# Down projections of the later pairs with the weights stationary and 512 tokens moving

## The chip, the cores and the metric

The kernel runs on one core of a Trainium2 chip. The metric is device time in microseconds (us), from the runs of the whole program; a profiled execution gives the span, from the first to the last instruction, and the times of each engine: PE (the matrix engine, with weight loads shown apart as PEld), DVE (vector), ACT (scalar), POOL (GpSimd) and SP (which here only issues DMAs).

## The reference

Chunked attention over 4 x 768 tokens gives x with 3072 rows of 512. Then come two feed-forward layers:

```python
def _moe_ref(x, w_a, w_b, w_out):
    a = x @ w_a
    b = x @ w_b
    return (a * b @ w_out).astype(np.float32)

def _moe2_ref(x, w_gate, w1, w2):
    logits = x @ w_gate
    P = np.exp(logits - logits.max())
    for _ in range(8):
        P /= P.sum(1, keepdims=True) + 1e-09
        P /= P.sum(0, keepdims=True) + 1e-09
        P *= N / E
    for e in range(E):
        h = np.maximum(x @ w1[e], 0.0)
        out += P[:, e:e + 1] * (h @ w2[e])
```

N is 3072 tokens, D 512, E 8 experts, w1[e] is 512 x 1024. The gate P is never negative. All data is float32.

## The kernel before, in words

Matmuls run in the fp32r format. Each operand is split into a high part and the rest (the low part), and three matmuls (high x high, high x low, low x high; PARTS) make one float32 product. Activations lie transposed in Y: 128 rows of the model dimension, 4 blocks of them, and the tokens along the free dimension.

Tokens are worked in 3 pairs of two 512-token blocks. The second layer's hidden units are cut into 32 slices of 256, so a pair has 32 units; u counts units over the pairs, 0 to 95, and the later pairs are u = 32 to 95 (k = u - 32). In each unit the up projection (x @ w1) is one 2 x 2 block product by Strassen's method in Winograd's form: 7 products (up(), L891, pos 0 to 6) of 6 matmuls each, 512 tokens moving. Its four results meet as sums: ACT copies a partial sum from PSUM (copy_u, copy_v, L1237 and L1241), DVE adds (sum_22, sum_21, L1515 and L1520).

The first pair's down projection (down(), L968) is plain: 8 groups of 6 matmuls, 512 columns. For the later pairs the down projection is itself a Winograd product (down_product(), L994, q = 0 to 6; DOWN gives for each q the operand H, the block of W2 and the PSUM pair). The hidden block is cut into A11, A12, A21, A22 (tokens by hidden units). ACT applies Relu to each (L1397, L1407, L1413, L1419), POOL makes the four sums S1 to S4 (hidden_sum(), L748 to L760), ACT makes the high parts of the seven operands (hidden_hi(), L1363) and POOL their low parts (hidden_lo(), L765). In down_product() H is the stationary operand and W2 moves, 256 columns at a time: 12 matmuls per q and unit. DVE adds each 128 x 256 result to Y, times the token's gate, which is a scalar of the partition (add_blocks(), L1580), so from then on Y of these pairs holds tokens along the partitions.

PE alternates: up(u, 0), down_product(u - 1, 0), up(u, 1), down_product(u - 1, 1) and so on. The order on each engine is written out by hand in one loop per engine, and each engine runs its list strictly in order. The waits are on semaphores: h_lo (low parts done), z_acc (adds done, which frees PSUM), c_ba (ACT's copy of product 0 into the other PSUM pair, L1370), r_rl (Relu done). SP loads per unit the blocks of W2 (fetch_blocks(), L514 and L515, double buffered) and W1 (fetch_up(), L491, double buffered), and stores the middle pair's 8 tiles in unit 67 (store(), L525). At the start of each pair the seven operands X of the up products are built from Y by ACT (L1191), DVE (L1475 to L1489) and POOL (L683) between the rest.

## Time and profile before

| | us |
|---|---|
| runs | 2695.83, 2698.10, 2700.66 (median 2698.1) |
| profiled execution | 2698.84 |
| its span | 2697.1 |
| PE busy | 2620.4 (97%) |
| POOL busy | 1578.0 (59%) |
| DVE busy | 1501.9 (56%) |
| ACT busy | 1121.4 (42%) |

The chain of work that ended last lies on PE for 89% of the span: 44% on L891, 23% on L994, 18% on L968. Busy time of PE is the time in which a matmul was under way; matmuls overlap, so what one costs is the distance of the starts in the timeline, not the duration shown. Idle time of another engine only costs where PE waits for it.

### The profile page before, as it was taken

The numbers are of one execution on the slowest core, as the hardware profiler recorded it, in microseconds if no ns is written. First come the engines' busy times: TensorE is split into PE (matmuls) and PEld (weight loads), VectorE is DVE, ScalarE is ACT, GpSimd is POOL, SyncE is SP. The second block draws the span as 40 slices with busy tenths as digits, with TensorE's granted clock in tenths as the row PEclk, the third lists the DMA queues.
The fourth block names the chain that finished last, engine by engine and source line by source line (L and its number), as shares of the span: only waits on it lengthen the run. The fifth ranks groups of instructions, "written<-read, shape, count | busy, mean of one in ns | idle before, by whom it ended". The sixth has DMA issues, their size and how long they took to land.

```text
span 2697.1 us, 44988 instructions
## 1 busy us (share of the span) xinstructions
PE 2620.4 (97%) x17568; PEld 2260.8 (84%) x17568; DVE 1501.9 (56%) x2807; ACT 1121.4 (42%) x1957; POOL 1578.0 (59%) x1304
## 2 busy tenths in 40 slices
PE   7879999999999999999999999999999999999999
PEld 6668878878777888888888999999998999999998
DVE  3454454454558555555565555555556555555555
ACT  4544332232333343343344444444445444444443
POOL 0045520010276777777766776767769767677676
PEclk9989999999999999999999999999999999999999
DMA  7746544334355666656646554554544645445453
GB/s 173 164 145 223 200 186 157 152 140 158 132 222 200 245 228 260 253 223 257 258 195 237 188 211 170 192 191 173 210 165 169 242 167 196 187 172 211 165 207 126
DMA packets 184498, 522.37 MB, mean 194 GB/s; under 512 B 55264, under 2 KB 119520, under 8 KB 165088
## 3 DMA queue, kind: packets, MB, share of 16 engines
q1 hardware_dynamic: 184288, 519.50, 52.8%
q8 instruction: 140, 2.29, 0.3%
q14 instruction: 70, 0.57, 0.1%
HBM read 359.02 MB, written 160.50 MB: 193 GB/s over the span
## 4 chain that ended last, share of the span: by engine, by line
PE 89%; DVE 4%; POOL 2%; issue 2%; ACT 1%; DMA 1%; SPq 1%; POOLq 0%; DVEq 0%; ACTq 0%
PE bank L891 44%; PE bank L994 23%; PE bank L968 18%; PE bank L814 2%; POOL X L683 1%; PE bank L853 1%; DVE tmp L1523 1%; PE bank L829 1%; POOL H L765 0%; DMA W<-w_kept 0%; PE bank L841 0%; DMA Qr<-in_q_dram 0%; DVE hid L1700 0%; ACT X L1191 0%; DVE Y L1475 0%
## 5 line engine op out<-in xcount | busy, mean ns | idle before, releaser
L891 PE MATMUL bank<-X,W 128*128 128x512 f32 x5550 | 1413.0, 393 | 18.6 <-ACT tmp L1241 5.8
L891 PEld LDWEIGHTS bank<-X,W 128*128 128x128 f32 x5550 | 1015.3, 189 | 219.5 <-issue 22.5
L1580 DVE SCALAR_TENSOR_TENSOR Y<-bank,gate,Y 128x256 f32<-128x256 f32 x1504 | 623.1, 477 | 413.4 <-PE bank L994 411.9
L994 PEld LDWEIGHTS bank<-W2n,H 128*128 128x128 f32 x5376 | 703.0, 191 | 43.0 <-POOL H L765 4.1
L994 PE MATMUL bank<-W2n,H 128*128 128x256 f32 x5376 | 714.9, 283 | 4.9 <-ACT bank L1370 2.4
L765 POOL TENSOR_TENSOR H<-tmp,H 128x512 fp32r<-128x512 f32 x352 | 452.5, 1307 | 129.1 <-ACT H L1363 129.1
L968 PE MATMUL bank<-W,hid 128*128 128x512 f32 x1536 | 387.1, 390 | 1.8 <-DVE Y L1553 1.8
L968 PEld LDWEIGHTS bank<-W,hid 128*128 128x128 f32 x1536 | 288.7, 188 | 62.1 <-DVE Y L1553 2.2
L1363 ACT ACTIVATE H<-tmp 128x512 fp32r<-128x512 f32 x352 | 212.0, 628 | 221.0 <-POOL tmp L760 127.1
L683 POOL TENSOR_TENSOR X<-Y,X 128x1024 fp32r<-128x1024 f32 x30 | 77.1, 2573 | 385.3 <-ACT X L1191 385.2
L1553 DVE SCALAR_TENSOR_TENSOR Y<-bank,gate,Y 128x512 f32<-128x512 f32 x224 | 166.9, 747 | 167.4 <-PE bank L968 166.4
L968 PE MATMUL bank<-hid,W 128*128 128x512 f32 x864 | 219.4, 389 | 1.2 <-issue 1.2
L1237 ACT ACTIVATE tmp<-bank 128x512 f32<-128x512 f32 x132 | 78.8, 597 | 280.1 <-PE bank L891 280.1
L968 PEld LDWEIGHTS bank<-hid,W 128*128 128x128 f32 x864 | 162.4, 188 | 35.4 <-issue 1.6
L1556 DVE TENSOR_TENSOR Y<-Y,bank 128x512 f32<-128x512 f32 x144 | 98.3, 684 | 155.7 <-PE bank L968 155.6
L646 POOL TENSOR_TENSOR W<-Ws,W 128x512 fp32r<-128x512 f32 x88 | 113.1, 1306 | 105.7 <-ACT W L1162 105.7
L1226 ACT ACTIVATE bank<-bank 128x512 f32<-128x512 f32 x131 | 75.9, 579 | 148.2 <-PE bank L891 148.2
L1515 DVE TENSOR_TENSOR tmp<-bank,tmp 128x512 f32<-128x512 f32 x100 | 69.1, 691 | 118.7 <-ACT tmp L1241 118.5
L1241 ACT ACTIVATE tmp<-bank 128x512 f32<-128x512 f32 x100 | 59.7, 597 | 174.4 <-PE bank L891 174.4
L646 POOL TENSOR_TENSOR W<-raw,W 128x512 fp32r<-128x512 f32 x88 | 88.6, 1026 | 72.8 <-ACT W L1162 72.8
L765 POOL TENSOR_TENSOR H<-ex,H 128x512 fp32r<-128x512 f32 x96 | 125.9, 1312 | 0.0
L1520 DVE TENSOR_TENSOR tmp<-bank,tmp 128x512 f32<-128x512 f32 x132 | 91.2, 691 | 46.7 <-PE bank L891 45.4
(113 smaller groups left out, 2270.7 us busy)
## 6 DMA issues: line engine op xcount, KB each, us to landing
W<-w_kept SPq DMA_DIRECT2D x88, 1792.0 KB, 11.1
W2n<-w2n_kept SPq DMA_DIRECT2D x64, 1536.0 KB, 7.4
w_kept<-W SPq DMA_DIRECT2D x44, 1792.0 KB, 8.1
raw<-in_moe_w_dram SPq DMA_DIRECT2D x64, 512.0 KB, 4.4
w2n_kept<-W SPq DMA_DIRECT2D x32, 1024.0 KB, 7.9
w2n_kept<-tmp SPq DMA_DIRECT2D x64, 512.0 KB, 8.0
W2n<-w2n_kept SPq DMA_DIRECT2D x64, 256.0 KB, 3.0
W<-w_kept SPq DMA_DIRECT2D x12, 1024.0 KB, 9.1
```

The costliest lines, as they stand in the source:

```text
L646: nc.gpsimd.tensor_tensor(w_piece(c, n, 1), w_piece_of(slot, n), w_piece(c, n, 0).bitcast(F32), ALU.subtract).then_inc(w1_lo, 1)
L683: nc.gpsimd.tensor_tensor(X[:, pos, 1], x_source(p, pos), X[:, pos, 0].bitcast(F32), ALU.subtract).then_inc(x_lo, 1)
L765: nc.gpsimd.tensor_tensor(H[:, pos, 1], of, H[:, pos, 0].bitcast(F32), ALU.subtract).then_inc(h_lo, 1)
L891: last = nc.tensor.matmul(into[:, :], W1[:, c % 2, ws, w_slot, kc, :], X[:, pos, xs, kc, :], start=(start and kc == 0 and n == 0), stop=(k ...
L968: last = nc.tensor.matmul(into[:, :], lhsT, rhs, start=(j == 0 and n == 0), stop=(j == 1 and n == 2))
L994: last = nc.tensor.matmul(ps[:, m * D // 2:(m + 1) * D // 2], H[:, h, a, at:at + P], W2n[k % 2][:, b, blk, :], start=(q in (0, 5) and m == ...
L1237: nc.scalar.activation(into, bank[BANK_B][:, :], ACT.Copy).then_inc(c_u, 1)
L1363: nc.scalar.activation(H[:, pos, 0], of, ACT.Copy).then_inc(h_hi, 1)
L1520: nc.vector.tensor_tensor(into, bank[BANK_E][:, :], of, ALU.add).then_inc(c_21, 1)
L1553: nc.vector.scalar_tensor_tensor(out=y, in0=ps, scalar=by, in1=y, op0=ALU.mult, op1=ALU.add).then_inc(y_acc, 1)
L1556: nc.vector.tensor_tensor(y, y, ps, ALU.add).then_inc(y_acc, 1)
L1580: nc.vector.scalar_tensor_tensor(out=y, in0=ps, scalar=by, in1=y, op0=ALU.mult, op1=ALU.add).then_inc(z_acc, 1)
```

## The change

The down product of the later pairs is transposed. A block of W2 (128 hidden units by 128 model columns) is now the stationary operand, and H moves with 512 tokens: 6 matmuls of 512 columns per q where there were 12 of 256. The result has the model dimension along the partitions and tokens along the free dimension. So the gate is no longer a scalar of the partition and can't be applied as the result is added. It is multiplied in first: gated() on DVE takes the maximum with zero and multiplies with gt, the expert's gates of the pair's 1024 tokens, repeated on all partitions; the four Relu passes on ACT go. gt (it takes the place of ex) is loaded every 4 units from g_rows in DRAM, which is written in unit 8 of the first pair from gates that PE transposes in unit 6. The adds into Y are 12 of 128 x 512 per unit, with no gate. The Winograd roles are swapped: the sums S are made of W2's blocks (block_sums, as many operations as before) and the T sums of the hidden blocks. DOWN and the orders H_HI and H_LO change with it, and V_N has one buffer where VN_AT had two. At the end the output tiles are turned back: 4 transposes on PE per 128-token tile (transpose_out()), a copy by ACT into the same place of Y (copy_out()), and the store, which now moves 512-byte pieces. For the middle pair this is done in units 65 to 68 and stored in unit 71; for the last pair it comes after the last product.

```diff
-DOWN = ((0, 0, 1), (1, 5, 1), (2, 3, 1), (4, 1, 0), (5, 2, 1), (6, 4, 0), (3, 6, 0))
-H_HI = (0, 2, 1, 4, 6, 3, 5)
-H_LO = (0, 1, 2, 4, 6, 5, 3)
+DOWN = ((0, 0, 1), (3, 5, 1), (2, 3, 1), (4, 1, 0), (1, 6, 1), (5, 4, 0), (6, 2, 0))
+H_HI = (0, 1, 2, 3, 4, 5, 6)
+H_LO = (0, 1, 3, 2, 4, 5, 6)
...
+            def load_gates(u):
+                p, e = u // V2, u % V2 // UE
+                if u == V2:
+                    sp.wait_ge(s_gw, 32)
+                    sp.wait_ge(p_down, NG * (M1 + V2 - 1))
+                else:
+                    sp.wait_ge(r_g, 4 * (u - V2))
+                of = g_rows[e, p * NG:(p + 1) * NG].rearrange("n t -> (n t)")
+                sp.dma_start(gt[:, :], of.unsqueeze(0).to_broadcast([P, PT_N])).then_inc(s_gt, 16)
...
-                    for m in range(2):
-                        at = (2 * half + m) * P
-                        for n, (a, b) in enumerate(PARTS):
-                            last = nc.tensor.matmul(ps[:, m * D // 2:(m + 1) * D // 2], H[:, h, a, at:at + P],
-                                                    W2n[k % 2][:, b, blk, :],
+                    for n, (a, b) in enumerate(PARTS):
+                        last = nc.tensor.matmul(b_half[pair][half][:, :],
+                                                W2n[k % 2][:, a, blk, half * P:(half + 1) * P], H[:, h, b, :],
+                                                start=(q in (0, 5) and n == 0), stop=(n == 2), skip_group_check=True)
                     last.then_inc(p_half, 1)
...
+            def transpose_out(p, i, into):
+                pe.wait_ge(z_acc, 12 * (p * V2 - 1) + (10 if i < SUB else 12))
+                if p == 1 and i > 0:
+                    pe.wait_ge(o_cp, i)
+                of = out_block(p, OUT_TILES[i])
+                for c in range(KC):
+                    last = nc.tensor.transpose(into[:, c * P:(c + 1) * P], of[:, c, :], ident[:, :])
+                last.then_inc(o_tr, 1)
...
+            def copy_out(p, i, of):
+                act.wait_ge(o_tr, NG * (p - 1) + i + 1)
+                nc.scalar.activation(out_block(p, OUT_TILES[i]), of[:, :].rearrange("p (c n) -> p c n", c=KC),
+                                     ACT.Copy).then_inc(o_cp, 1)
...
-                    if i == 0 and first:
-                        nc.vector.tensor_scalar(y, ps, by, None, ALU.mult).then_inc(z_acc, 1)
+                    if i == 0 and q < 5:
+                        nc.vector.tensor_copy(y, ps).then_inc(z_acc, 1)
                     else:
-                        nc.vector.scalar_tensor_tensor(out=y, in0=ps, scalar=by, in1=y, op0=ALU.mult,
-                                                       op1=ALU.add).then_inc(z_acc, 1)
+                        nc.vector.tensor_tensor(y, y, ps, ALU.add).then_inc(z_acc, 1)
+            def gated(u, n):
+                ...
+                nc.vector.scalar_tensor_tensor(out=into, in0=of, scalar=0.0, in1=gt[:, l * TB:(l + 1) * TB],
+                                               op0=ALU.max, op1=ALU.mult).then_inc(r_g, 1)
```

On DVE, in a unit of the last pair, before: from the adds of product 4 (banks 5 and 6) over those of product 5 (banks 3 and 4) to sum_21; the sum_22 stands first.

```order
L1515 TENSOR_TENSOR ex<-bank2,ex 128x512 [waits c_v,p_prod]
L1580 SCALAR_TENSOR_TENSOR Y<-bank5,gate,Y 128x256 [waits p_half]
L1580 SCALAR_TENSOR_TENSOR Y<-bank5,gate,Y 128x256
L1580 SCALAR_TENSOR_TENSOR Y<-bank6,gate,Y 128x256 [waits p_half]
L1580 SCALAR_TENSOR_TENSOR Y<-bank6,gate,Y 128x256
L1580 SCALAR_TENSOR_TENSOR Y<-bank3,gate,Y 128x256 [waits p_half]
L1580 SCALAR_TENSOR_TENSOR Y<-bank3,gate,Y 128x256
L1580 SCALAR_TENSOR_TENSOR Y<-bank4,gate,Y 128x256 [waits p_half]
L1580 SCALAR_TENSOR_TENSOR Y<-bank4,gate,Y 128x256
L1520 TENSOR_TENSOR tmp<-bank2,tmp 128x512 [waits c_u,p_prod]
```

The same place of the changed program, where gt holds the gates:

```order
L1587 TENSOR_TENSOR tmp<-bank2,tmp 128x512 [waits c_v,p_prod]
L1678 SCALAR_TENSOR_TENSOR tmp<-tmp,gt 128x512 [waits c_22]
L1648 TENSOR_TENSOR Y<-Y,bank5 128x512 [waits p_half]
L1648 TENSOR_TENSOR Y<-Y,bank6 128x512 [waits p_half]
L1678 SCALAR_TENSOR_TENSOR tmp<-bank1,gt 128x512 [waits h_lo,p_prod]
L1648 TENSOR_TENSOR Y<-Y,bank3 128x512 [waits p_half]
L1648 TENSOR_TENSOR Y<-Y,bank4 128x512 [waits p_half]
L1592 TENSOR_TENSOR tmp<-bank2,tmp 128x512 [waits c_u,p_prod]
L1678 SCALAR_TENSOR_TENSOR tmp<-tmp,gt 128x512 [waits c_21]
```

Two gate multiplications now stand between the sum of V and the adds of product 5 (banks 3 and 4), and a third follows sum_21.

On PE, the end of the changed program: the last down product (banks 3 and 4), which waits for the adds of the product before it, and the first transposes of output tiles.

```order
L1039 MATMUL bank3<-H,W2n1 128x512 [waits z_acc,h_lo]
L1039 MATMUL bank3<-H,W2n1 128x512 x2
L1039 MATMUL bank4<-H,W2n1 128x512 [waits z_acc]
L1039 MATMUL bank4<-H,W2n1 128x512 x2
L1060 MATMUL bank0<-ident,Y 128x128 [waits z_acc]
L1060 MATMUL bank0<-ident,Y 128x128 x3
L1060 MATMUL bank1<-ident,Y 128x128 [waits z_acc]
L1060 MATMUL bank1<-ident,Y 128x128 x3
```

Before, the program of PE ended with the product, and the store waited for DVE's last adds alone; now eight tiles of four transposes follow, each into a bank of its own.

On POOL, one unit of the program before, and one of the changed program; L748, L754, L756 and L760 (after: L800, L803, L805, L809) are the four sums, L765 (L813) the low parts.

```order
L748 TENSOR_TENSOR tmp<-tmp 128x512 [waits r_rl]
L754 TENSOR_TENSOR ex<-tmp 128x512 [waits h_sum]
L756 TENSOR_TENSOR tmp<-tmp 128x512
L765 TENSOR_TENSOR H<-ex,H 128x512 [waits h_hi]
L765 TENSOR_TENSOR H<-tmp,H 128x512 [waits h_hi] x2
L760 TENSOR_TENSOR tmp<-tmp,ex 128x512 [waits r_rl,h_sum]
```

```order
L800 TENSOR_TENSOR tmp<-tmp 128x512 [waits r_g]
L803 TENSOR_TENSOR tmp<-tmp 128x512 [waits h_sum]
L805 TENSOR_TENSOR tmp<-tmp 128x512
L813 TENSOR_TENSOR H<-tmp,H 128x512 [waits h_hi] x3
L809 TENSOR_TENSOR tmp<-tmp 128x512 [waits r_g,h_sum]
L813 TENSOR_TENSOR H<-tmp,H 128x512 [waits h_hi] x4
```

The number of operations is the same. Two low parts (of products 0 and 4) now stand ahead of the sums where one stood; the first low part behind the sums is that of product 1 in both.

## Rows read from the trace of the kernel before

**Rows 1.** The page's busy us and share of the span by engine.

```profile
PE 2620.4 (97%) x17568; PEld 2260.8 (84%) x17568; DVE 1501.9 (56%) x2807; ACT 1121.4 (42%) x1957; POOL 1578.0 (59%) x1304
```

**Rows 2.** Costliest groups: xcount, busy us, mean ns, idle before and its releaser.

```profile
L891 PE MATMUL bank<-X,W 128*128 128x512 f32 x5550 | 1413.0, 393 | 18.6 <-ACT tmp L1241 5.8
...
L994 PE MATMUL bank<-W2n,H 128*128 128x256 f32 x5376 | 714.9, 283 | 4.9 <-ACT bank L1370 2.4
```

**Rows 3.** Busy time by stretch: us and instructions by engine, clock, DMA share, GB/s.

```profile
1440.00:1980.00 540.00, 540.00 (x3451) 490.89 (x3450) 308.05 (x713) 251.40 (x437) 377.43 (x299) 1.00 0.51 188
...
1000.00:1380.00 380.00, 380.00 (x1678) 314.67 (x1677) 214.47 (x260) 149.38 (x243) 285.87 (x261) 1.00 0.64 244
```

**Rows 4.** Timeline: start, us, engine, line; first pair, then later pairs, PE.

```profile
1203.01 1.52 PE L968 MATMUL bank<-W,hid 128*128 128x512 f32 x6
...
1204.37 1.52 PE L891 MATMUL bank<-X,W 128*128 128x512 f32 x6
...
2008.23 1.55 PE L891 MATMUL bank<-X,W 128*128 128x512 f32 x6
...
2011.05 1.55 PE L891 MATMUL bank<-X,W 128*128 128x512 f32 x6
```

**Rows 5.** Timeline of one steady unit of the later pairs.

```profile
2013.87 1.55 PE L891 MATMUL bank<-X,W 128*128 128x512 f32 x6
...
2015.52 0.60 ACT L1241 ACTIVATE tmp<-bank 128x512 f32<-128x512 f32 x1 [1.62 <-PE bank L891]
...
2016.22 0.69 DVE L1515 TENSOR_TENSOR tmp<-bank,tmp 128x512 f32<-128x512 f32 x1 [1.21 <-ACT tmp L1241]
...
2016.83 1.65 DVE L1580 SCALAR_TENSOR_TENSOR Y<-bank,gate,Y 128x256 f32<-128x256 f32 x4
...
2018.96 1.29 POOL L748 TENSOR_TENSOR tmp<-tmp 128x512 f32<-128x512 f32 x1 [3.68 <-ACT tmp L1413]
...
2020.33 1.29 POOL L754 TENSOR_TENSOR ex<-tmp 128x512 f32<-128x512 f32 x1
```

**Rows 6.** By form: count, min/median/max ns, first and last start; L1700 and L1556.

```profile
L1700 DVE SCALAR_TENSOR_TENSOR hid<-tmp,hid x64: 682/1343/2414, 752.5 to 1408.9; 128x512 fp32r<-128x512 f32 x64
...
L1556 DVE TENSOR_TENSOR Y<-Y,bank x144: 669/686/689, 239.7 to 856.2; 128x512 f32<-128x512 f32 x144
```

**Rows 7.** Timeline: four transposes on PE in the attention.

```profile
163.82 0.87 PEld L863 LDWEIGHTS bank<-ident,On 128*128 128x128 f32 x4
...
167.28 0.42 PEld L841 LDWEIGHTS bank<-ident,Pr 128*128 128x128 f32 x4
...
181.99 0.60 PE L863 MATMUL bank<-ident,On 128*128 128x128 f32 x4
```

**Rows 8.** Timeline: PE's stalls at the two pair starts.

```profile
1430.03 1.65 PE L891 MATMUL bank<-X,W 128*128 128x512 f32 x6 [1.69 <-DMA W<-w_kept]
...
2037.78 1.67 PE L891 MATMUL bank<-X,W 128*128 128x512 f32 x6 [1.19 <-ACT ex L1241]
...
2049.21 1.49 PEld L994 LDWEIGHTS bank<-W2n,H 128*128 128x128 f32 x12 [1.61 <-POOL H L765]
```

**Rows 9.** SP's issues about unit 67, landing times there, DMA rate in 0:9.

```profile
2113.99 0.41 SPq L491 DMA_DIRECT2D W<-w_kept  x1
...
2126.94 0.53 SPq L514 DMA_DIRECT2D W2n<-w2n_kept  x1
...
W<-w_kept SPq DMA_DIRECT2D x1, 1792.0 KB, 12.3
...
GB/s 0 0 0 0 0 0 0 0 46 123 46 32 125 241 341 353 346 346 334 318 323 257 291 289 296 294 260 152 62 8 0 26 10 0 26 10 0 32 5 0
```

**Rows 10.** Timeline at the end, landing of the last stores, L525's first and last start.

```profile
2678.03 3.03 PE L994 MATMUL bank<-W2n,H 128*128 128x256 f32 x24
...
2682.27 1.67 PE L994 MATMUL bank<-W2n,H 128*128 128x256 f32 x12 [1.21 <-ACT bank L1370]
...
out_dram<-Y SPq DMA_DIRECT2D x8, 256.0 KB, 2.4
...
L525 SPq DMA_DIRECT2D out_dram<-Y x24: 332/476/873, 1471.0 to 2694.0; - x24
```

More of the change, by code:

```diff
@@ L241, in build @@
         z_acc = sem("z_acc")
+        g_tr = sem("g_tr")
+        g_row = sem("g_row")
+        s_gw = sem("s_gw")
+        s_gt = sem("s_gt")
+        o_tr = sem("o_tr")
+        o_cp = sem("o_cp")
         s_wg = sem("s_wg")
@@ L606, in _ @@
                     fetch_up(C1 + u)
+                if u % UE == 0:
+                    load_gates(u)
                 fetch_blocks(u)
-                if u % V2 == 3:
-                    store(u // V2 - 1)
+                if u == V2 + 3:
+                    store(0)
+                if u == 2 * V2 + 7:
+                    store(1)
             store(PAIRS - 1)
@@ L659, in block_sums @@
                 w = M1 + u
-                b = b_blocks(w)
-                b11, b12, b21, b22 = (b[:, i] for i in range(4))
-                t1, t3, t2, t4 = (T_SUMS[:, i] for i in range(4))
+                b = w2_blocks(w)
+                a11, a21, a12, a22 = (b[:, i] for i in range(4))
+                s1, s3, s2, s4 = (S_SUMS[:, i] for i in range(4))
                 pool.wait_ge(s_raw[item_w2(w) % 2], 16 * (item_w2(w) // 2 + 1))
@@ L1089, in _ @@
                         total(TOTALS.index((u, pos)))
+                    if u == 6 and pos == 0:
+                        transpose_gates()
+                    if (u, pos) in OUT_SLOTS:
+                        transpose_out(1, OUT_SLOTS.index((u, pos)), b_gate)
                 if u <= V2:
@@ L1093, in _ @@
                 down_product(M2 - 1, q)
+            for i in range(NG):
+                transpose_out(2, i, bank[OUT_BANKS[i]])
         @block.scalar
@@ L1387, in _ @@
                 else:
-                    act.wait_ge(h_lo, NP * (k - 2) + H_LO.index(5) + 1)
-                copy_u(c, a12)
-                act.wait_ge(p_prod, NP * c + 4)
+                    act.wait_ge(h_lo, NP * (k - 1))
+                copy_u(c, b21)
+                if k > 0:
+                    hidden_hi(k - 1, 6)
+                hidden_hi(k, 0)
+                if n is not None:
+                    operand_hi(n, p, 1, c)
                 if k == 0:
@@ L1416, in _ @@
                 hidden_hi(k, 2)
-                hidden_hi(k, 1)
-                act.wait_ge(c_21, c + 1)
-                nc.scalar.activation(a12, a12, ACT.Relu).then_inc(r_rl, 1)
+                hidden_hi(k, 3)
                 hidden_hi(k, 4)
-                hidden_hi(k, 6)
-                hidden_hi(k, 3)
                 if n is not None:
@@ L1426, in _ @@
             hidden_hi(M2 - V2 - 1, 5)
+            hidden_hi(M2 - V2 - 1, 6)
+            for i in range(NG):
+                copy_out(2, i, bank[OUT_BANKS[i]])
         @block.vector
@@ L1562, in add_blocks @@
                 p, i = unit_of(M1 + u)
-                l, dh, first = {1: (1, 0, True), 2: (1, 1, True), 3: (0, 0, True), 4: (0, 1, True),
-                                5: (1, 1, False), 6: (1, 0, False)}[q]
-                for m in range(SUB):
-                    n = l * SUB + m
-                    at = p * PT_N + n % 2 * TB + dh * D // 2
-                    y = Y[:, n // 2, at:at + D // 2]
-                    ps = b_half[DOWN[q][2]][m // 2][:, m % 2 * D // 2:(m % 2 + 1) * D // 2]
-                    by = gate[:, p * NG + n, i // UE:i // UE + 1]
-                    if m % 2 == 0:
-                        dve.wait_ge(p_half, 2 * NP * k + 2 * q + m // 2 + 1)
-                    if i == 0 and q == 1 and m == 0:
+                dh, l = added(q)
```

209 lines of the change are left out of this document (134 added, 75 removed).

## The prediction

> **What bounds the kernel now.** I read the busy shares first. PE is busy 2620 of 2697 us [rows 1], so the matmul stream is the bound, and the question is what one matmul costs and where the stream stops. The list of costliest groups shows two kinds of matmul: the 512-column ones of the up products (L891), and the 5376 of L994 with 256 columns, which the change turns into half as many of 512 [rows 2]. The busy times by stretch show PE without a gap over 1440 to 1980 and over 1000 to 1380, at a granted clock of 1.00, which is the 2.4 GHz level [rows 3]. The timeline then prices a slot. In the second layer's first pair, where every matmul has 512 columns, a group of 6 takes 1.36 us (1203.01 to 1204.37), so a slot of an up product and a down group is 2.72 us. In the later pairs the slot of 6 x 512 and 12 x 256 is 2.82 us (2008.23 to 2011.05) [rows 4]. A unit there has 7 slots, 19.74 us. The idle rows of DVE, ACT and POOL in that stretch are all inside PE's cover.
>
> **The steady units.** A slot falls from 2.82 to 2 x 1.36 = 2.72 us, if 512 moving columns of H cost what 512 of hid cost. That is 0.10 us a slot and 0.70 us a unit. The 64 units of later pairs have 63 whose down products stand beside an up chain (the first of them still runs the old down(), the last products stand alone): 63 x 0.70 = **-44.2 us**. Bounds: if a 256-column matmul is worth exactly half a 512-column one, 0; if the 12 small ones carry all of what lies above 7 x 1.36, that is the 44 already taken, so 44 is also the upper end.
>
> The same row against a rule: per slot, twelve 256-column matmuls take 2.82 - 1.36 = 1.46 us, 122 ns each, and 512 columns take 227 ns. The Trainium skill (TensorE: Matmul & The Clock Gate, section "Back-to-back issue gap") gives the isolated gap as columns over 2.4 plus 2.5 ns. By that rule joining two matmuls saves 2.5 ns, some 7 us in all, and the change would not pay for its transposes. The trace disagrees, with 17 ns saved a pair; I go by the trace, and the rule is a rival below.
>
> **Does the rest keep up with a 19.04 us unit?** I count from the start of a unit's up product 0. Up product i starts at 2.72 i, down product q at 2.72 q + 1.36, and an engine that waits for a product starts about 1.6 us after the product's start (2013.87 on PE to 2015.52 on ACT [rows 5]).
>
> DVE now has 12 adds of 512 (0.686 each, [rows 6]) instead of 24 scaled adds of 256 (0.415 apart: 1.65 for 4, [rows 5]), and four gate multiplications of about 0.7: 8.2 + 2.8 + 1.4 = 12.4 us of 19.04, where it was 11.3 of 19.74. ACT loses four Relu passes. POOL keeps 11 operations of 1.25 to 1.3, about 14.5 us. None is full, so only latency can hurt, at two places.
> (a) The sixth add. Up product 4 starts at 10.88, ACT's copy ends at 13.13, the sum of V starts at 13.23 (2015.52 and 2016.22 in [rows 5], shifted). Then, in DVE's order, come the gate multiplication of V, two adds, the gate multiplication of the next block and the first add of product 5, which PE's product 6 waits for. Starts lie 0.61 apart where the next is ready (2016.22 to 2016.83), so: 13.95, 14.6, 15.2, 15.8, 16.45, done 17.15. PE loads the weights for product 6 at 17.46. Margin 0.3 us, or zero with full durations of 0.69 to 0.75. I take no stall and keep 0.2 us a unit, 12 us in all, for the range.
> (b) POOL's chain. The multiplication of block B12 is done at 16.5. POOL makes three sums and the low part for product 1: first sum 16.65 (PE is 1.36 apart from it where it waits on itself: 2018.96 to 2020.33), then 18.0, 19.3, 20.55, done 21.85. PE wants it at 22.9. The last gate multiplication (at 18.65) has both operands in SBUF and falls on those sums. For such a pair the row shows what happens: hid<-tmp,hid takes 682 ns alone, 1343 in the median, 2414 at most, whereas adds from PSUM never leave 669 to 689 [rows 6]. So POOL comes up to 0.7 late, still in time by 0.35. No stall.
>
> The Trainium skill (VectorE: DVE Perf Modes, section "Two Vector instructions with no wait between them") says that the second SBUF input is read through an interface shared with GpSimd. The trace agrees in that only the form with two SBUF inputs stretches. Without this sharing (b) would have 1.05 us to spare instead of 0.35; the sum is the same either way.
>
> **What is added on PE's path.** Four 128-column transposes take 0.60 us of weight loads and matmuls (181.99 [rows 7]; bounds 0.42 and 0.87 by the weight loads of the other two rows). Eight tiles of the middle pair are transposed inside units 65 to 68: 8 x 0.6 = **+4.8**. ACT's eight copies sit in its idle time. The gates' two transposes in unit 6: **+0.3**.
>
> **Edges.** At the start of the later pairs PE waited 1.7 us for the reload of W1 (1430.03 [rows 8]). On SP the first load of the gate rows now stands ahead of it: one issue of 0.5 us (2126.94 [rows 9]) and 0.5 MB, at 350 GB/s 1.5 us: **+2.0** (0 to 4). The other 15 gate loads come in units with 5 us of slack on SP's queue; free. At the start of the last pair PE stalls twice: 1.2 us at 2037.78 (waiting for ACT) and 1.6 us at 2049.21 (waiting for POOL) [rows 8]. There ACT's copy of V now also stands behind the high part that waits for DVE's gate multiplication, and that stands behind a long operand sum: about 1.2 us more, and POOL's chain behind that 2 more: **+3** (0 to 7). The middle pair's eight stores move to unit 71 and go in 512-byte pieces; W1 behind them took 12.3 us to land from 2113.99, so until 2126.3; the next unit, which wants it, had begun just before SP's issue at 2126.94, which waits for the same end of unit [rows 9]. With the unit 0.7 shorter: **+1** (0 to 3). Pieces of 512 bytes moved at up to 353 GB/s at the start (the loads of K and Q), so they are not slow in themselves [rows 9].
>
> **The end.** Before, the last unit's product 0 started at 2679.5 (half way in the x24 row), product 1 at 2682.27 after a stall of 1.2 [rows 10], and the span ended 17.6 us after product 0. After: product 1 needs POOL's low part and starts 3.0 to 3.6 after product 0, then six products of 1.36 with two short waits end at 12.4. Eight transposed tiles at 0.6 follow one another to 17.2, ACT's last copy ends at 18.0, and a store needs 2.4 to land; before, the last was issued at 2694.0, landed at 2696.4 and stood 0.7 ahead of the span's end [rows 10]. That is 21.1; if the stores' 2 MB at 350 GB/s set the pace (13.7 + 6 + 1.5 + 0.7), 21.9. So **+4** (2 to 8).
>
> **Sum.** -44.2 + 4.8 + 0.3 + 2.0 + 3.0 + 1.0 + 4.0 = -29.1. The profiled execution took 2698.8 (span 2697.1 and 1.7 around it), the median of the runs is 2698.1. 2698.8 - 29.1 = 2669.7; I say **2670**.
>
> **Rivals.**
> 1. Thin margin (a) fails: the sixth add is late by up to 0.2 us and PE stalls in every unit. For it: full durations leave nothing. Against: back-to-back starts at 0.61. 63 x 0.2 = 12.6: 2682.
> 2. The edges cost their upper bounds (4 + 7 + 3 + 8 instead of 10): +12, 2682. For it: five things meet at the pair start. Chance as below.
> 3. The slower side: DVE and POOL hold each other. If both gate multiplications with two SBUF inputs cost DVE their median instead of 0.68, (a) is late by 0.66 - 0.3 = 0.36; if POOL also loses 0.7 twice, (b) is late by 0.35. Together 0.71 a unit, 45 us: 2715. It decides from 29.1 / 63 = 0.46 us of stall a unit. Against: the first of the two falls where POOL waits (12.5 to 15.3), so it is free of that.
> 4. The slot doesn't shrink (the skill's rule above): -44 goes, the costs stay. 2698.8 + 15.1 = 2714, with the rule's 7 us 2707. Against: rows 4, on the same operand types.
>
> **Chances.** The forecast with its own spread 0.60, rival 1 0.16, rival 2 0.14, rival 3 0.06, rival 4 0.04. The range of 8 in 10 reaches from 2660 (edges at their lower bounds: -10) to 2688 (rivals 1 and 2 partly together). 0.2% is 5.4 us, about what a measurement of this kernel can tell from no change. Slower by more: rivals 3 and 4, most of it, 0.08; within: 0.02; faster: 0.90.
>
> **What would show it.** After: 512-column groups 1.36 us apart in the later pairs, 2688 matmuls instead of 5376, PE without idle over a steady stretch, unit 19.04. Step (a) is wrong if PE idles before product 6 for DVE; step (b) if it idles before product 1 for POOL; the edge terms if the wait for W1 at the first pair start isn't near 3.7 us and the stalls at the second not near 3 us more than before. The prediction fails outright if the slot stays at 2.82 or if PE idles over 0.46 us in each unit.

## The result, and the profile after

| us | median | lowest to highest | runs |
|---|---|---|---|
| before | 2699.38 | 2695.83 to 2700.84 | 4 |
| after | 2675.49 | 2671.34 to 2677.47 | 4 |

The ratio is 0.9911, with a 95% interval of 0.9894 to 0.9929. The change takes 23.9 us off the median. The profiled execution took 2671.34 us (span 2669.6), which is 27.5 less than before's; 3.3 of that has nothing to do with the change, as the landmarks below show.

The page of the changed kernel: first the busy times, then its two kinds of matmul in the list of costliest groups, which answer to [rows 1, 2].

```profile
PE 2586.2 (97%) x14946; PEld 2128.0 (80%) x14946; DVE 1570.4 (59%) x2295; ACT 994.2 (37%) x1718; POOL 1610.1 (60%) x1304
...
L940 PE MATMUL bank<-X,W 128*128 128x512 f32 x5550 | 1403.8, 391 | 22.8 <-ACT tmp L1310 9.6
...
L1039 PE MATMUL bank<-H,W2n 128*128 128x512 f32 x2688 | 682.8, 390 | 7.7 <-DVE Y L1648 4.1
```

5376 matmuls of 256 columns are 2688 of 512. The busy times by stretch (us and instructions of PE, PEld, DVE, ACT and POOL, granted clock, DMA share, GB/s), where the first row answers to the first of [rows 3]:

```profile
1440.00:1980.00 540.00, 540.00 (x2384) 447.08 (x2383) 349.15 (x513) 199.98 (x339) 405.66 (x311) 1.00 0.54 202
...
1400.00:1440.00 40.00, 35.27 (x145) 27.72 (x145) 25.99 (x30) 13.28 (x20) 26.80 (x16) 0.96 0.61 223
2020.00:2080.00 60.00, 54.36 (x236) 43.66 (x235) 42.03 (x54) 25.23 (x41) 51.34 (x36) 0.97 0.48 176
```

PE has no idle time in the steady stretch. DVE has 41 us more to do there than before and ACT 51 less, and both are still far from full. The two short rows are the pair starts, where PE is idle and the clock is below 1.00. The timeline of PE in the steady stretch (start, duration, engine, line), against [rows 4]:

```profile
1960.45 1.52 PE L940 MATMUL bank<-X,W 128*128 128x512 f32 x6
1961.81 1.52 PE L1039 MATMUL bank<-H,W2n 128*128 128x512 f32 x6
1963.17 1.52 PE L940 MATMUL bank<-X,W 128*128 128x512 f32 x6
```

Each group of six starts 1.36 us after the one before. A slot is 2.72 us and a unit of seven slots 19.04.

**Where the time went, by landmarks.** The attention and the first pair, which the change hardly touches, vary by up to 9 us between executions (with the same code there, landmark A lies at 1409.57 to 1418.65), so I count from landmarks of PE. A is the down group of unit 32 that waits 1.8 us for DVE in both kernels (1414.39 before, 1411.12 after). T33, T63, T65 and T95 are the starts of product 0 of the up chains of units 33, 63, 65 and 95: at 1430.03, 2022.33, 2067.47 and 2659.73 before, at 1429.85, 2001.25, 2049.85 and 2627.44 after.

| stretch (us) | before | after | after less before | of it steady slots | the rest |
|---|---|---|---|---|---|
| A to T33 | 15.64 | 18.73 | +3.1 | | +3.1 |
| T33 to T63, 30 units | 592.30 | 571.40 | -20.9 | -21.1 | +0.2 |
| T63 to T65 | 45.14 | 48.60 | +3.5 | -1.4 | +4.9 |
| T65 to T95, 30 units | 592.26 | 577.59 | -14.7 | -21.1 | +6.4 |
| T95 to the end | 37.37 | 42.16 | +4.8 | -0.7 | +5.5 |
| A to the end | 1282.71 | 1258.48 | **-24.2** | -44.2 | +20.0 |

A second execution of the changed kernel gives 1258.25 from A to the end, although its A lies 7.5 us later (1418.65). In these two executions the kernel repeats within 0.3 us from A on, and -24.2 agrees with the medians. Single stretches repeat less well: x2_noturn below has one with the same instructions that is 2.3 us longer, and of the kernel before there is one profile alone.

### The profile page after: what moved, and what is told of

Its sections match the earlier page's. It is cut to its first block, busy times and chain, and to the rows that moved or that the text cites. A ratio compares the mean times of both kernels' runs of the same rounds, so it can differ in the third digit from the quotient of the medians.

```text
span 2669.6 us, 39021 instructions
## 1 busy us (share of the span) xinstructions
PE 2586.2 (97%) x14946; PEld 2128.0 (80%) x14946; DVE 1570.4 (59%) x2295; ACT 994.2 (37%) x1718; POOL 1610.1 (60%) x1304
## 4 chain that ended last, share of the span: by engine, by line
PE 87%; DVE 4%; POOL 3%; issue 2%; DMA 1%; ACT 1%; SPq 1%; ACTq 0%; DVEq 0%; POOLq 0%
PE bank L940 43%; PE bank L1039 21%; PE bank L1017 19%; PE bank L863 2%; POOL X L735 1%; DMA W<-w_kept 1%; POOL H L813 1%; PE bank L902 1%; DVE tmp L1595 1%; PE bank L878 1%; SPq L570 0%; PE bank L890 0%; ACT X L1260 0%; DMA Qr<-in_q_dram 0%; DVE hid L1798 0%
## 5 line engine op out<-in xcount | busy, mean ns | idle before, releaser
L940 PEld LDWEIGHTS bank<-X,W 128*128 128x128 f32 x5550 | 1043.5, 189 | 250.9 <-issue 23.6
L813 POOL TENSOR_TENSOR H<-tmp,H 128x512 fp32r<-128x512 f32 x448 | 577.0, 1300 | 295.4 <-ACT H L1435 293.4
L1039 PE MATMUL bank<-H,W2n 128*128 128x512 f32 x2688 | 682.8, 390 | 7.7 <-DVE Y L1648 4.1
L1648 DVE TENSOR_TENSOR Y<-Y,bank 128x512 f32<-128x512 f32 x752 | 497.1, 683 | 265.1 <-PE bank L1039 265.1
L1039 PEld LDWEIGHTS bank<-H,W2n 128*128 128x128 f32 x2688 | 504.2, 188 | 115.6 <-issue 7.0
L1435 ACT ACTIVATE H<-tmp 128x512 fp32r<-128x512 f32 x448 | 276.8, 630 | 475.1 <-DVE tmp L1678 248.3
L1306 ACT ACTIVATE tmp<-bank 128x512 f32<-128x512 f32 x132 | 79.1, 599 | 388.2 <-PE bank L940 388.2
L1587 DVE TENSOR_TENSOR tmp<-bank,tmp 128x512 f32<-128x512 f32 x132 | 91.3, 692 | 171.5 <-ACT tmp L1310 171.2
L1628 DVE TENSOR_TENSOR Y<-Y,bank 128x512 f32<-128x512 f32 x144 | 98.5, 685 | 158.7 <-PE bank L1017 158.6
L1310 ACT ACTIVATE tmp<-bank 128x512 f32<-128x512 f32 x132 | 78.8, 597 | 212.2 <-PE bank L940 124.9
L1678 DVE SCALAR_TENSOR_TENSOR tmp<-tmp,gt 128x512 f32<-128x512 f32 x128 | 125.2, 978 | 4.4
L1678 DVE SCALAR_TENSOR_TENSOR tmp<-bank,gt 128x512 f32<-128x512 f32 x128 | 88.0, 688 | 43.6 <-PE bank L940 42.5
```

The costliest lines, as they stand in the source:

```text
L813: nc.gpsimd.tensor_tensor(H[:, pos, 1], hidden_at(k, pos), H[:, pos, 0].bitcast(F32), ALU.subtract).then_inc(h_lo, 1)
L940: last = nc.tensor.matmul(into[:, :], W1[:, c % 2, ws, w_slot, kc, :], X[:, pos, xs, kc, :], start=(start and kc == 0 and n == 0), stop=(k ...
L1039: last = nc.tensor.matmul(b_half[pair][half][:, :], W2n[k % 2][:, a, blk, half * P:(half + 1) * P], H[:, h, b, :], start=(q in (0, 5) and ...
L1435: nc.scalar.activation(H[:, pos, 0], hidden_at(k, pos), ACT.Copy).then_inc(h_hi, 1)
L1587: nc.vector.tensor_tensor(into, bank[BANK_E][:, :], of, ALU.add).then_inc(c_22, 1)
L1628: nc.vector.tensor_tensor(y, y, ps, ALU.add).then_inc(y_acc, 1)
```

## The experiments

Each median below is of 4 or 5 runs, and its ratio is taken to runs of the kernel before on the same chip; x4_relu is a single run. The stretches between landmarks come from one profiled execution each.

### x1_narrow: the width alone

Each matmul of the down product is split in two halves of tokens. Weights, layout, gates and transposes stay as after.

```diff
+                    for m in range(2):
+                        at = m * TB // 2
...
-                                                W2n[k % 2][:, a, blk, half * P:(half + 1) * P], H[:, h, b, :],
+                                                    W2n[k % 2][:, a, blk, half * P:(half + 1) * P],
+                                                    H[:, h, b, at:at + TB // 2],
```

> The changed kernel, but each 512-token matmul of down_product() is issued as two of 256 tokens with the same stationary block, so there are 5376 again; all else (roles, gates, transposes, order) stays. Theory (the width of the moving operand is the whole gain): the slot of 6 x 512 and 12 x 256 goes back from 2.72 to 2.82 us, the unit from 19.04 to 19.74, 63 units x 0.70 = 44 us on the changed kernel's 2675.5: about 2719, slower than the kernel before by some 20. Rival (the new roles or the removed work make the gain): the slot stays at 2.72, about 2676.

Measured: 2716.39 us (2713.99 to 2717.56), ratio to before 1.007, interval 1.0053 to 1.0087. The timeline of PE in its steady stretch:

```profile
1961.95 1.55 PE L940 MATMUL bank<-X,W 128*128 128x512 f32 x6
1963.34 1.59 PE L1041 MATMUL bank<-H,W2n 128*128 128x256 f32 x12
1964.78 1.55 PE L940 MATMUL bank<-X,W 128*128 128x512 f32 x6
```

The slot is 2.83 again, and T33 to T95 takes 1237.56 us, 40.0 more than after. T33 to T63 alone takes 592.30, which is what it took before. The whole gain comes with the 512 columns; as each 256-column matmul has a weight load of its own, fewer weight loads and wider moving operands are one step here, and no run takes them apart. Without it the change is 20 us slower than before in the medians and 16.4 from A to the end (1299.09), and that is the price of all the rest.

### x3_one and x3_two: how much room the sixth add has

One or two more DVE adds of 128 x 512 stand ahead of product 5's adds in each unit; their results go to a buffer that nobody reads then.

```diff
+                    if q == 5 and half == 0 and u < M2 - 1:
...
+                        for _ in range(1):
+                            nc.vector.tensor_tensor((lg[:, :], hid1[:, 0, 0, 0, :])[_], y, ps, ALU.add)
```

> The changed kernel with one more DVE add of 128 x 512 (PSUM and SBUF in, a scratch tile out) in each unit, just ahead of the adds of product 5. In the trace the add that PE's product 6 waits for ends some 0.4 us ahead of PE's weight load. Theory of margins: one add is 0.6 us, so PE stalls 0.2 us a unit, 61 units: 12 us, about 2688. Rival (the margin is wider than the trace seems to say, since PE's order has other slack): no change, 2676. Rival (there is no margin at all): 37 us, 2713.

> As x3_one, with two such adds in each unit. Theory of margins: 1.2 - 0.4 = 0.8 us a unit, 61 units: 49 us, about 2724. Together with the run with one add it gives the slope (0.6 us of PE time per added add) and where it begins. Rival (wider margin): under 20 us, below 2696.

Measured: one add 2684.8 us (2683.85 to 2686.64), ratio 0.9955, interval 0.9941 to 0.997; two adds 2721.36 (2717.1 to 2723.46), ratio 1.0088, interval 1.0073 to 1.0103. T33 to T95 grows by 12.5 and 50.4 us, 0.20 and 0.81 in each of 62 units. With one add the timeline shows the wait on the weight load (DVE and PE of one unit):

```profile
1968.34 0.68 DVE L1649 TENSOR_TENSOR lg<-Y,bank 128x512 f32<-128x512 f32 x1
1968.93 1.28 DVE L1653 TENSOR_TENSOR Y<-Y,bank 128x512 f32<-128x512 f32 x2
1969.73 1.22 PEld L1039 LDWEIGHTS bank<-H,W2n 128*128 128x128 f32 x6 [0.33 <-issue]
```

With two, PE's row names DVE:

```profile
1964.43 0.68 DVE L1649 TENSOR_TENSOR lg<-Y,bank 128x512 f32<-128x512 f32 x1
1965.03 0.68 DVE L1649 TENSOR_TENSOR hid<-Y,bank 128x512 fp32r<-128x512 f32 x1
1965.62 1.28 DVE L1653 TENSOR_TENSOR Y<-Y,bank 128x512 f32<-128x512 f32 x2
...
1966.45 1.63 PE L1039 MATMUL bank<-H,W2n 128*128 128x512 f32 x6 [0.53 <-DVE Y L1653]
```

The second add cost 0.61 a unit, the distance of DVE's starts, so the path is full by then. The first cost 0.20, so 0.4 us of it was covered. That is the margin of the sixth add, and it is what the timeline of after shows (DVE and PE around product 6, in unit 95):

```profile
2622.35 0.69 DVE L1678 SCALAR_TENSOR_TENSOR tmp<-tmp,gt 128x512 f32<-128x512 f32 x1
2622.95 1.28 DVE L1648 TENSOR_TENSOR Y<-Y,bank 128x512 f32<-128x512 f32 x2
...
2624.15 0.68 DVE L1678 SCALAR_TENSOR_TENSOR tmp<-bank,gt 128x512 f32<-128x512 f32 x1
...
2624.75 1.27 DVE L1648 TENSOR_TENSOR Y<-Y,bank 128x512 f32<-128x512 f32 x2
...
2625.86 1.32 PEld L1039 LDWEIGHTS bank<-H,W2n 128*128 128x128 f32 x6
```

The first of the two adds at 2624.75 ends near 2625.43, and the weights load at 2625.86.

### x4_relu: one SBUF input where two gate multiplications had two

The second and fourth gate multiplication of a unit only take the maximum with zero, with one SBUF input. Their gates are left out of the result.

```diff
+                if n in (1, 3):
+                    nc.vector.tensor_scalar(into, of, 0.0, None, ALU.max).then_inc(r_g, 1)
```

> The changed kernel, but the second and fourth gate multiplication of each unit (both operands in SBUF) are a maximum with zero alone: the gate is left out of two of the four blocks. Theory: those two stretch to 0.98 us in the mean and make POOL's third sum 1.75 long instead of 1.29, but PE never waits for either in the steady units, so POOL's sum goes back to 1.29 and units 33 to 62 stay at 19.04 us; only the pair start, where all is late, may lose 1 to 2 us. Rival (the shared access to SBUF costs PE time): the steady unit gets shorter than 19.04 or the time falls by over 3 us.

Measured: one run, 2668.16 us; T33 to T95 1196.23 against 1197.59 and 1197.62 after. DVE and POOL in the steady stretch of x4_relu:

```profile
1981.14 0.72 DVE L1679 TENSOR_SCALAR tmp<-tmp 128x512 f32<-128x512 f32 x1
1981.53 1.49 POOL L805 TENSOR_TENSOR tmp<-tmp 128x512 f32<-128x512 f32 x1
```

The same place of the kernel after, with POOL's low parts behind it:

```profile
2627.01 1.24 DVE L1678 SCALAR_TENSOR_TENSOR tmp<-tmp,gt 128x512 f32<-128x512 f32 x1
...
2627.66 1.75 POOL L805 TENSOR_TENSOR tmp<-tmp 128x512 f32<-128x512 f32 x1
...
2629.37 3.78 POOL L813 TENSOR_TENSOR H<-tmp,H 128x512 fp32r<-128x512 f32 x3
...
2631.30 1.32 PEld L1039 LDWEIGHTS bank<-H,W2n 128*128 128x128 f32 x6
```

The contention is real. After, it makes DVE's operation 1.24 long instead of 0.69 (2622.35) and POOL's third sum 1.75 instead of 1.29 (2018.96 in [rows 5]). x4_relu halved it and did not remove it: its operation takes 0.43 where POOL is idle (1976.48) and 0.72 here, and POOL's sum came down to 1.49 and not to the expected 1.29. But the contention costs PE nothing in a steady unit. PE has no idle time there with it, the low part of product 1 ends near 2630.65 (a third of the row at 2629.37), and its weights load at 2631.30, 0.65 later; with half of it gone the slot is still 2.72. T33 to T95 is 1.4 us less, all of it behind T63. The total of the single run is 7.3 us below the median of the kernel after, more than the 3 us that the rival was to show, but from A to the end it takes 1256.34, which is only 2.1 less.

### x2_noturn: no turning back

The transposes and ACT's copies go, and Y's blocks are stored as they stand, in rows of 2 KB. The output of the later pairs is not turned back.

```diff
-                if (u, pos) in OUT_SLOTS:
-                        transpose_out(1, OUT_SLOTS.index((u, pos)), b_gate)
...
-            for i in range(NG):
-                transpose_out(2, i, bank[OUT_BANKS[i]])
...
+                        sp.dma_start(out_d[p * NG + i], Y[:, 2 * dh + half, at:at + TB]).then_inc(s_out, 16)
```

> The changed kernel without turning the output back: the 64 transposes of output tiles and ACT's 16 copies are left out, and Y is stored as it lies, transposed, in 2 KB rows. Theory: the transposes cost 0.60 us a tile on PE inside units 65 to 68 (4.8 us), the end is 5.5 us longer than before's by transposes, copies and 512-byte stores, and the wait for W1 behind the stores of unit 71 costs 1.5: together 10 to 12 us less than the changed kernel's 2675.5: about 2664 to 2666. Rival (PE would have waited for DVE and POOL at these places anyway, and the stores cost the same in 2 KB rows): 5 us less, 2671.

Measured: 2661.47 us (2660.54 to 2664.58), ratio 0.987, interval 0.9855 to 0.9885. A to the end takes 1247.57, which is 10.9 less than after and within the 10 to 12 of the theory; the medians differ by 14.0. T95 to the end takes 34.85 instead of 42.16 (-7.3), T33 to T95 1194.02 instead of 1197.59 (-3.6). The price of the middle pair's tiles is in PE's timeline of the kernel after:

```profile
2062.26 1.52 PE L940 MATMUL bank<-X,W 128*128 128x512 f32 x6
...
2064.99 0.60 PE L1060 MATMUL bank<-ident,Y 128*128 128x128 f32 x4
...
2068.19 1.52 PE L940 MATMUL bank<-X,W 128*128 128x512 f32 x6
```

From 2062.26 to 2068.19 it is 5.93 us where two slots take 5.44, so a tile adds 0.49, and eight add 3.9. T65 to T95 falls by 5.8: these 3.9, 0.9 in unit 72, where PE waits 0.25 for W1 instead of 1.19, and 1.0 in unit 65, where a wait for POOL is gone. But T63 to T65, where both kernels have the same instructions, takes 50.91 instead of 48.60. Its waits are 0.6 shorter in all, and three groups ran at the lower clock where one did after. So 2 us of such a stretch can come from the clock alone. Two of the three groups (PE in x2_noturn; from start to start they take 2.70 and 2.56):

```profile
2033.63 2.90 PE L1040 MATMUL bank<-H,W2n 128*128 128x512 f32 x6 [2.74 <-ACT bank L1439]
2036.33 2.77 PE L941 MATMUL bank<-X,W 128*128 128x512 f32 x6
```

### f1_pair: the order at the pair starts

At the last pair's start PE stalls in unit 63 and 64 of the kernel after (PE's rows with a wait, and the two behind the 2.85; against the second and third of [rows 8]):

```profile
2018.00 1.65 PE L940 MATMUL bank<-X,W 128*128 128x512 f32 x6 [2.71 <-ACT tmp L1310]
...
2025.22 1.88 PE L1039 MATMUL bank<-H,W2n 128*128 128x512 f32 x6 [2.85 <-DVE Y L1648]
2026.90 2.77 PE L940 MATMUL bank<-X,W 128*128 128x512 f32 x6
2029.46 1.70 PE L1039 MATMUL bank<-H,W2n 128*128 128x512 f32 x6
...
2033.63 1.63 PE L1039 MATMUL bank<-H,W2n 128*128 128x512 f32 x6 [1.11 <-ACT bank L1442]
...
2037.52 1.61 PE L1039 MATMUL bank<-H,W2n 128*128 128x512 f32 x6 [0.91 <-DVE Y L1648]
```

The 2.71 is ACT's copy of V, which stands behind two operations that wait for DVE. f1_pair puts the copy ahead of them, and DVE's third operand sum behind product 5's adds.

```diff
-                hidden_hi(k, 0)
-                if n is not None:
-                    operand_hi(n, p, 1, c)
-
+                if n is None and k > 0:
+                    hidden_hi(k, 0)
...
                 copy_v(c, V_N)
+                if n is not None or k == 0:
+                    hidden_hi(k, 0)
+                if n is not None:
+                    operand_hi(n, p, 1, c)
...
-                if n is not None:
-                    operand_sum(n, p, 2)
                 gated(u, 2)
                 add_blocks(u - 1, 5)
+                if n is not None:
+                    operand_sum(n, p, 2)
```

> The changed kernel itself, unedited, for a comparison on one chip with the runs beside it: 2671 to 2677 again; both theories of the other runs count from it.

> Order only, in units 32 and 63, where the operands of the next pair are built: ACT copies V (copy_v) ahead of the high part of product 0 and of the X operand, which wait for DVE; in unit 63 DVE does the third gate multiplication and the adds of product 5 ahead of the third operand sum. Theory (PE's waits of 2.7 and 2.9 us in unit 63 and 1.2 in unit 32 are an order of queues, not work): all three go, some of it comes back in unit 64: 3 to 6 us less than the changed kernel. Rival (DVE and POOL are simply full there, five big operations more in a unit): the wait moves to product 1 or 2 of the next unit, within 1 us of the changed kernel.

Measured: the kernel after once more 2674.36 us (2671.15 to 2678.65), ratio 0.9917, interval 0.9902 to 0.9932; f1_pair 2669.04 (2664.73 to 2672.2), ratio 0.9896, interval 0.9876 to 0.9916. The medians differ by 5.3 us, and the intervals overlap. Of the profiled executions of this pair, 2678.65 and 2668.40, 9.1 of the 10.3 us between them lie ahead of A (1418.65 and 1409.57): from A to the end f1_pair takes 1257.13, only 1.1 to 1.3 less than the kernel after. PE's waits in f1_pair, at the first start and at the second:

```profile
1428.07 2.93 PE L940 MATMUL bank<-X,W 128*128 128x512 f32 x6 [2.97 <-DMA W<-w_kept]
```

```profile
2020.56 1.62 PE L1039 MATMUL bank<-H,W2n 128*128 128x512 f32 x6 [1.41 <-DVE Y L1650]
2030.17 2.90 PE L1039 MATMUL bank<-H,W2n 128*128 128x512 f32 x6 [3.90 <-ACT bank L1442]
```

The stall of 2.71 went, and waits of 1.41 and 3.90 stand there instead. The waits between T63 and T65 fall from 7.6 to 5.3 us, but two groups behind the 3.90 run at the lower clock where one did, and T63 to T65 takes 46.80 instead of 48.60. So the order was a part only. That the rest moved to product 1 of the next unit, as the rival says, fits a backlog: the sum of the work that must be done at a pair start is what is late.

### f3_sp: the loads and stores on SP's queue

The gate load moves into unit 31, and the middle pair's stores are split over units 71 and 73.

```diff
+                if u == V2 - 1:
+                    load_gates(V2)
                 keep_t_lo(u)
...
                 if u == 2 * V2 + 7:
-                    store(1)
+                    store(1, range(4))
+                if u == 2 * V2 + 9:
+                    store(1, range(4, NG))
```

> Order on SP only: the first load of gate rows is issued ahead of the store of the last low parts (some 9 us earlier) and not behind it, and the middle pair's eight stores go four in unit 71 and four in unit 73. Theory: the 1.8 us wait for W1 at the start of unit 33 shrinks by the 1 to 2 us that the gate load took of the queue, DVE's wait for the gates (1.1) goes, and the 1.2 us wait at unit 72 goes: 2 to 4 us less. Rival (W1's landing is set by the bandwidth of all that is asked for there, not by its place behind the gates): 1.2 us less, unit 72 alone.

Measured: 2672.14 us (2666.39 to 2674.96), ratio 0.9905, interval 0.9888 to 0.9923; A to the end 1256.02, so -2.4. At the first start the order on SP of the kernel after, and PE's wait:

```profile
1413.10 0.38 SPq L552 DMA_DIRECT2D gt<-g_rows  x1
...
1415.11 0.54 SPq L517 DMA_DIRECT2D W<-w_kept  x1
...
1429.85 1.67 PE L940 MATMUL bank<-X,W 128*128 128x512 f32 x6 [1.79 <-DMA W<-w_kept]
```

From A to W1's issue it is 3.99 us (3.42 in f3_sp, 3.43 before), and from the issue to T33 14.74 (12.21 before). In f3_sp, T33 comes 15.56 after A with no wait for W1, and before it came 15.64 after A. So the +3.1 up to T33 is W1 behind the gate load, 0.6 in the issue and 2.5 in the landing. That PE also waits 1.17 for ACT and runs a group at the lower clock before it is hidden by W1: f1_pair took the 1.17 away, and T33 came at 18.50 instead of 18.48 to 18.73. But f3_sp then has its first down product wait 1.30 for DVE (1432.97), which takes 1.3 us of it back. Counted from A to T63 and against before less its 21.1 of steady slots, the kernel after is 3.3 us longer, f3_sp 2.2, and f4_all and f4_again, which have the order of f1_pair too, 0.4 and 0.0. It took both changes to clear the first start.

At the stores, SP of the kernel after:

```profile
2170.40 11.59 SPq L570 DMA_DIRECT2D out_dram<-Y  x8
2182.09 0.59 SPq L517 DMA_DIRECT2D W<-w_kept  x1
```

The same place of the kernel before, in unit 67, where the eight stores moved 2 KB rows:

```profile
2108.43 5.46 SPq L525 DMA_DIRECT2D out_dram<-Y  x8
```

The eight issues occupied SP for 11.6 us instead of 5.5, and W1 was issued only at 2182.09 (in the unit before, 0.71 behind the second W2 load). PE waited 1.19 for it at 2189.39. Split in two, that wait is gone.

### f4_all, f4_again and f5_all: put together

f4_all is f1_pair and f3_sp with one thing more: ACT's last eight copies go to scratch buffers in which a tile's row is contiguous, and the last stores move 2 KB pieces.

```diff
+        def out_tile(i):
+            if i < 4:
+                return raw[:, i // 2, i % 2 * TB:(i % 2 + 1) * TB]
...
+                            sp.dma_start(out_d[p * NG + n], out_tile(i)).then_inc(s_out, 16)
```

> Both of these, and at the end ACT's copies of the last pair's turned tiles go to contiguous scratch (raw, Ws, gt), so that the last stores move 2 KB rows and not 512-byte pieces. In the trace of the changed kernel the last stores run at 287 GB/s, those of the kernel before at 380. Theory: 2.1 MB at 380 instead of 287 is 1.8 us less at the end; with the 5 to 10 of the other two it gives 2665 to 2669. Rival (the end is set by transposes and copies, which take 4.0 us for eight tiles, not by the stores): nothing from the end, 2669 to 2672.

> The version with the three mends (pair order, SP order, 2 KB stores at the end) once more, to compare on one chip with the run beside it: 2665 to 2670.

f5_all also takes the last adds of unit 62 ahead of DVE's operand work for product 3 and 4, which moves to unit 64.

```diff
+                if first_use(w) is not None:
+                    operand_lo(first_use(w), p - 1, 3)
+                    operand_sum(first_use(w), p - 1, 4)
...
-                if n is not None:
-                    operand_lo(n, p, 3)
-                    operand_sum(n, p, 4)
```

> As f4_again, and DVE does the last adds of unit 62's products ahead of the low part of X 3 and the fourth operand sum (both move from the end of unit 63 into unit 64). In the traces PE's product 1 of unit 64 waits 2.7 to 3.9 us for ACT's copy of product 0, which waits for those adds. Theory (order again): that wait shrinks by about 2.5 us, 2665 less 2.5 against its neighbour. Rival (what is taken here appears at up products 3 and 6 of unit 64, which need the operands that are now later): under 1 us.

| | median us | ratio to before | interval | A to the end | T95 to the end |
|---|---|---|---|---|---|
| f4_all | 2667.47 | 0.9891 | 0.9875 to 0.9907 | 1250.13 | 39.98 |
| f4_again | 2664.53 | 0.9868 | 0.9854 to 0.9883 | 1249.74 | 40.00 |
| f5_all | 2664.39 | 0.9871 | 0.9853 to 0.9889 | 1251.56 | 40.02 |

f4 is faster than both kernels: 8.1 to 8.7 us less than the kernel after from A to the end, and 6.9 less in the median of f4_all, on the same chip as the second run of the kernel after (their intervals still overlap by 0.0005; that of f4_again, on another chip, lies below that of the kernel after). The end gained 2.2 of it, the stretch from A to T63 2.9 to 3.3. The busy times by stretch while the last stores move, of the kernel after and of f4_all (last columns: share of the DMA engines' time, GB/s):

```profile
2664.00:2667.00 3.00, 0.00 (x0) 0.00 (x0) 0.00 (x0) 0.00 (x0) 0.00 (x0) 0.62 0.99 286
```

```profile
2661.00:2664.00 3.00, 0.28 (x3) 0.04 (x1) 0.00 (x0) 1.29 (x3) 0.00 (x0) 1.00 1.03 380
```

The DMA engines are busy all the time in both, so it is the rate that differs, and not how fast SP issues.

f5_all gained nothing over f4. The wait it was to shorten became one for POOL:

```profile
2027.21 1.87 PE L1053 MATMUL bank<-H,W2n 128*128 128x512 f32 x6 [3.75 <-POOL H L827]
```

## Why the prediction was right, and where its terms were off

The forecast was 2670 and the median is 2675.5; the range held it. The mechanism is the one that was predicted, and no rival took its place.

| term | predicted | measured | shown by |
|---|---|---|---|
| steady units | -44.2 | -44.0 | T33 to T63 (-20.9 in 30 units), x1_narrow |
| gates' transposes | +0.3 | not told apart | lies ahead of A |
| first pair start | +2.0 | +3.1 | f3_sp, f1_pair |
| last pair start | +3.0 | +4.9 | T63 to T65 |
| middle pair's transposes | +4.8 | +3.9 | distances of starts, x2_noturn |
| stores and W1 in unit 72 | +1.0 | +1.4 | f3_sp (T71 to T72: 20.40 after, 19.04 there) |
| T65 to T95, what is left | | +1.1 | the wait for POOL at 2054.85 |
| end | +4.0 | +5.5 | x2_noturn, f4_all |
| sum | -29.1 | -24.1 | |

- **The slot.** 1.36 us a group was predicted from the 512-column matmuls of the first pair, and measured in all steady units. By the Trainium skill's rule for an isolated matmul (TensorE: Matmul & The Clock Gate, "Back-to-back issue gap") the wider matmuls would have saved 7 us in all, less than the edges cost. x1_narrow shows that the split into 256 columns alone costs 40 us in 62 units: 0.70 in each steady unit, and less where PE waits anyway. Rival 4 is out.
- **Margin (a).** Predicted 0.3 us; the trace shows 0.43 and the added adds 0.4. Rival 1 did not come, but the two experiments show that its mechanism is there: 0.2 us beyond the margin costs 12.5 us.
- **Margin (b).** Predicted 0.35 under contention, measured 0.65, since POOL lost 0.4 to 0.5 and not 0.7. Among the gate multiplications the form that stretches is the one that was named. But two SBUF inputs aren't needed for it, as the prediction had it: in x4_relu an operation with one stretched from 0.43 to 0.72. The groups of the gate multiplication after (duration min/median/max in ns):

```profile
L1678 DVE SCALAR_TENSOR_TENSOR tmp<-bank,gt x128: 677/685/692, 1419.0 to 2643.2; 128x512 f32<-128x512 f32 x128
L1678 DVE SCALAR_TENSOR_TENSOR tmp<-tmp,gt x128: 691/812/2003, 1421.7 to 2646.0; 128x512 f32<-128x512 f32 x128
```

Rival 3 took the median of hid<-tmp,hid, 1343 [rows 6], for both of these in a unit. The one on the path of (a) takes 0.69 (2622.35), since POOL is idle beside it, as the prediction said against the rival; the one behind it takes 1.24 (2627.01). PE has no idle time in the steady stretch, so neither costs it anything.
- **Edges.** This is where the forecast is off. Rival 2 was right in its direction, and with 5 of its 12 us: every edge came out dearer than its single value and inside its own bounds, +20.0 in all (with the middle pair's transposes) where 14.8 was said. The weak step is to have priced each edge by one late thing. At the first start, the queue took what was said (0.5 and 1.5) and 1 us more to land. At the last start the sum said ACT 1.2 and POOL 2 more. PE in fact waited 2.71 for ACT (1.19 before), 1.5 more, and then 2.85 for DVE at a product that didn't wait before. Before's later waits (1.21 at 2049.24, 1.54 at 2053.84, 0.61 at 2058.94) became shorter, 1.11 and 0.91. In all the waits are 7.6 us where they were 4.55, which is 3.0 of the 4.9; 1.5 is the lower clock (0.3 in the group at 2025.22, 1.2 in that at 2026.90). So no single wait grew as was said, and the clock wasn't in the sum. In f1_pair and f5_all a wait came up elsewhere when one was shortened, which fits one backlog.
- **The middle pair's transposes** were priced by the length of a row of four, 0.60 [rows 7]. The next group overlaps that row, and the distance of starts grows by only 0.49. What this saved was spent by a wait that the prediction didn't have: unit 65 still pays for the pair start, with 0.77 us for POOL's low part (2054.85 against 2052.57 + 1.36, and 0.14 more until the next start).
- **The wait for W1 at the first start** was to be 3.7 and is 1.79. By its own sign the term would be wrong, and yet T33 came 3.1 later, because other waits stood ahead of it and hid in it: a wait's length in the trace isn't its price.
- **The end.** By its own steps, after product 0 of the last products (2646.48): the products end at 12.45 (predicted 12.4), the transposes at 16.1 (17.2), ACT's last copy at 17.1 (18.0), the span at 23.1 (21.1 or 21.9). Everything up to the stores was early, and the stores ate it. PE, ACT and SP at the end, against [rows 10]:

```profile
2657.47 1.63 PE L1039 MATMUL bank<-H,W2n 128*128 128x512 f32 x6 [0.19 <-DVE Y L1648]
...
2658.93 3.66 PE L1060 MATMUL bank<-ident,Y 128*128 128x128 f32 x32
2659.57 4.03 ACT L1446 ACTIVATE Y<-bank 128x512 f32<-128x512 f32 x8 [5.49 <-PE bank L1060]
2660.19 6.28 SPq L570 DMA_DIRECT2D out_dram<-Y  x8
```

The assumption that failed was the rate, and with it the landing: the last store took 3.6 us from issue to landing, not 2.4. The rate was taken from loads in 512-byte pieces at up to 353 GB/s [rows 9]; these stores in 512-byte pieces move at 286, and those in 2 KB pieces at 380 for a while.

- **Readings and sums of the prediction that don't hold.** The stall of 1.6 us at 2049.21 is idle time of the weight loads; PE's own row there shows 1.21, for ACT. The stalls at 2053.84 and 2058.94 were not counted. 63 x 0.70 is 44.1. The lower bounds of the edges take 8 off, and 9.4 with the tiles at 0.42, not 10. The sums change little by it, 0.1 us in the forecast and 0.6 to 2 at the lower end of the range.

Of what the forecast missed by, the edges are 4.9 us. The middle pair's transposes were 0.9 too dear and the wait of 1.1 in unit 65 was missing, and that these two cancel is luck.

What stays open: how much of the 3.0 us of longer waits at the last start is POOL and DVE holding each other, and how much the longer queue on DVE. No run takes these apart.

## What to carry to other kernels

On a kernel that one engine bounds, price the steady unit by the distance of starts of the same shape elsewhere in the same trace, and then check the slack of each engine that hands over within the unit, by its order of work: here 0.4 us was the difference between a gain and, two adds later, a loss. Price the edges by their whole backlog (all the work that must be done before the pair's first products), not by the one instruction that the trace names as late; moving that one gave back 1.8 us of 4.9 there, and 1.1 to 1.3 in all. Take a DMA's rate from transfers in its own direction and piece size, and keep a large load's place in the issue queue: eight stores in 512-byte pieces ahead of it held it for 11.6 us.
